# A gated linear-attention and MLP kernel on one core: the scores move onto two 64-row tiles of TensorE, the state update alternates column halves, and k is loaded without its zeroed half

## The reference

```
m_new = max(f + m, i);  f_stab = exp(f + m - m_new);  i_stab = exp(i - m_new)
C = f_stab * C + i_stab * outer(v, k)      # 40 x 40 state per head
n = f_stab * n + i_stab * k
y = sigmoid(o) * (C q) / max(|n . q|, 1)
```

```
h  = relu(x^T @ w_tok1) @ w_tok2;  u = x + h^T
x2 = u + relu(u @ w_ch1) @ w_ch2                 # 320 -> 1536 -> 320
out = (sigmoid(conv5(x2)) * (x2 @ w_val)) @ w_out
```

## Time and profile before

| | us |
|---|---|
| median of three runs | 288.86 |
| profiled execution, whole | 291.4 |
| its span, first to last instruction | 289.3 |
| TensorE busy | 264.7 (91%) |
| VectorE busy | 180.0 (62%) |
| ScalarE busy | 115.4 (40%) |
| GpSimd busy | 85.7 (30%) |

### The profile page before, as it was taken

How to read it: one execution, slowest core, us unless ns; L and a number is a source line. 1 busy time by engine, 2 the same in 40 slices (tenths; PEclk the granted TensorE clock), 3 DMA queues, 4 the chain that set the end, 5 groups by cost and what they waited for, 6 DMA issues and landing times.

```text
span 289.3 us, 5204 instructions
## 1 busy us (share of the span) xinstructions
PE 264.7 (91%) x1964; PEld 247.3 (85%) x1964; DVE 180.0 (62%) x401; ACT 115.4 (40%) x212; POOL 85.7 (30%) x102
## 2 busy tenths in 40 slices
PE   0598788999999999999999999999999999999675
PEld 0587677679799999999999997899999999999564
DVE  7988877486878568535866303537653168742991
ACT  2664545488444432443432223322232332232731
POOL 4415578903654553155004000000040000130710
PEclk9999999999999999999999999999999999999988
DMA  7699987664765143220000010000000100000101
GB/s 219 155 274 321 302 265 219 212 198 124 208 189 132 57 142 91 84 68 3 0 0 2 3 66 2 0 0 2 0 2 23 45 1 2 0 2 0 56 13 68
DMA packets 26289, 25.68 MB, mean 89 GB/s; under 512 B 13977, under 2 KB 22009, under 8 KB 26265
## 3 DMA queue, kind: packets, MB, share of 16 engines
q1 hardware_dynamic: 21976, 18.72, 22.2%
q10 hardware_dynamic: 4288, 6.64, 7.1%
HBM read 23.34 MB, written 2.02 MB: 88 GB/s over the span
## 4 chain that ended last, share of the span: by engine, by line
PE 74%; DVE 7%; issue 7%; POOL 5%; ACT 4%; DMA 1%; SPq 0%; ACTq 0%; POOLq 0%; DVEq 0%
PE shared L1172 30%; PE h_ps L1306 22%; PE s_ps L1210 4%; PE hv_ps L1191 2%; PE s_ps L1244 2%; PE hv_ps L1195 2%; DVE gate L1039 2%; PE shared L1271 2%; PE h_ps L1244 2%; POOL qs L597 2%; PE shared L1221 1%; DMA mask_sb<-mask 1%; PE shared L1318 1%; DVE prob L930 1%; PE shared L1256 1%
## 5 line engine op out<-in xcount | busy, mean ns | idle before, releaser
L1104 DVE SCALAR_TENSOR_TENSOR h_lo<-shared,h_hi 128x384 fp32r<-128x384 f32 x48 | 26.5, 557 | 40.2 <-ACT h_hi L824 40.1
L1306 PE MATMUL h_ps<-ch_hi,h_hi 128*128 128x320 f32 x144 | 45.4, 315 | 0.0
L1306 PE MATMUL h_ps<-ch_hi,h_lo 128*128 128x320 f32 x144 | 44.5, 309 | 0.0
L824 ACT ACTIVATE h_hi<-shared 128x384 fp32r<-128x384 f32 x48 | 23.1, 488 | 53.2 <-PE shared L1172 50.1
L1306 PE MATMUL h_ps<-ch_lo,h_hi 128*128 128x320 f32 x144 | 44.3, 308 | 0.0
L1172 PE MATMUL shared<-u_hi,ch_hi 128*128 128x384 f32 x96 | 33.1, 344 | 0.1
L1172 PE MATMUL shared<-u_lo,ch_hi 128*128 128x384 f32 x96 | 32.6, 339 | 0.0
L1172 PE MATMUL shared<-u_hi,ch_lo 128*128 128x384 f32 x96 | 32.5, 339 | 0.0
L1210 PE MATMUL s_ps<-q_in,k_in 128*128 128x128 f32 x192 | 27.1, 300 | 3.9 <-DMA q_in<-qT 3.9
L1210 PEld LDWEIGHTS s_ps<-q_in,k_in 128*128 128x128 f32 x192 | 25.2, 211 | 6.1 <-DMA q_in<-qT 4.5
L1039 DVE SCALAR_TENSOR_TENSOR gate<-x,conv_sb,gate 128x384 f32<-128x384 f32 x44 | 29.0, 668 | 1.0
(11 more groups left out here) (181 smaller groups left out, 550.3 us busy)
## 6 DMA issues: line engine op xcount, KB each, us to landing
G_all<-G_scratch SPq DMA_DIRECT2D x11, 512.0 KB, 5.8
o_sig<-on ACTq DMA_DIRECT2D x2, 960.0 KB, 6.7
k_in<-kT SPq DMA_DIRECT2D x24, 80.0 KB
q_in<-qT SPq DMA_DIRECT2D x24, 80.0 KB
kn_in<-kn SPq DMA_DIRECT2D x12, 160.0 KB, 4.3
v_in<-vn SPq DMA_DIRECT2D x12, 160.0 KB, 4.8
stage<-ch ACTq DMA_DIRECT2D x3, 640.0 KB, 4.3
out<-o_sb SPq DMA_DIRECT2D x12, 160.0 KB, 1.8
```

The source lines that it names most:

```text
L824: act.activation(h_hi[i % 3][:], ps_of(key)[:, 0:T], ACT.Relu).then_inc(hi_ready, 1)
L1104: took(dve.scalar_tensor_tensor(out=h_lo[i % 3][:], in0=ps_of(key)[:, 0:T], scalar=0.0, in1=h_hi[i % 3][:].bitcast(F32), op0=ALU.max, op1= ...
L1306: last = pe.matmul(h2_ps[t][:, 0:DM], a[:, tile_cols(t)], w[:, f, :], start=(f == 0 and n == 0), stop=(f == FT - 1 and n == 2))
```

## The change

The scores lose the zeroed half: k_in becomes 128 x 512 like q_in, and a score matmul reads only its group's 40 rows (partitions 0 to 39 or 64 to 103) of k and q. The groups alternate, j outer and g inner, and each group still has its own bank. Both banks are now waited for at once, on TensorE before the first score matmul and on VectorE before the first product. The delta matmuls alternate between the output halves 0 to 63 and 64 to 103 in the same way. kn of the last chunk of a batch (u = 5 and 11), which nothing reads, is not loaded. The two memsets of k_in go, and the first k is issued before the wait for `zeroed`. Both k_in buffers now have room of their own, so k uses them in turn for all chunks.

```diff
-        k_in = [sb("k_in0", [P, 2, HG * L]), sb("k_in1", [P, 2, HG * L], at=a_at + 4 * S)]
+        k_in = [sb(f"k_in{k}", [P, HG * L]) for k in range(2)]
...
-        def k_buffer(u):
-
-            return 1 if u < NC and u % 2 else 0
-
-        def k_users(u):
-
-            return [x for x in range(u + 1) if k_buffer(x) == k_buffer(u)]
+        def kn_users(u):
+
+            return [x for x in range(u % 2, u + 1, 2) if x % NC < NC - 1]
...
             def k_chunk(u):
-                users = k_users(u)
-                if len(users) > 1:
-
-                    sp.wait_ge(s_ready, 2 * (users[-2] + 1))
+                if u >= 2:
+
+                    sp.wait_ge(s_ready, 2 * (u - 1))
                 for g in range(2):
-                    sp.dma_start(k_in[k_buffer(u)][64 * g:64 * g + D, g, :],
-                                 kT[u, g]).then_inc(k_loaded[k_buffer(u)], 16)
+                    sp.dma_start(k_in[u % 2][64 * g:64 * g + D, :], kT[u, g]).then_inc(k_loaded[u % 2], 16)
...
-                kn_chunk(u)
+                if u % NC < NC - 1:
+                    kn_chunk(u)
                 v_chunk(u)
...
-            sp.wait_ge(zeroed, 4)
             k_chunk(0)
+            sp.wait_ge(zeroed, 2)
             q_chunk(0)
...
-            pool.memset(k_in[1][:], 0.0).then_inc(zeroed, 1)
...
-            dve.memset(k_in[0][:], 0.0).then_inc(zeroed, 1)
...
                 if n < NC:
+                    dve.wait_ge(s_ready, 2 * u + 2)
                     for g in range(2):
                         w = 2 * u + g
                         dve.wait_ge(exp_ready, w + 1)
-                        dve.wait_ge(s_ready, w + 1)
                         dve.tensor_tensor(prob[w % 4][:], s_ps[g][:], prob[w % 4][:], ALU.mult).then_inc(prob_ready, 1)
...
-                    for g in range(2):
-                        w = 2 * u + g
-                        if w >= 2:
-                            pe.wait_ge(prob_ready, w - 1)
-                        for j in range(HG):
-                            last = pe.matmul(s_ps[g][:, tile_cols(j)], k_in[k_buffer(u)][:, g, tile_cols(j)],
-                                             q_in[k][:, tile_cols(j)], start=True, stop=True)
-                        last.then_inc(s_ready, 1)
+                    if u >= 1:
+                        pe.wait_ge(prob_ready, 2 * u)
+                    for j in range(HG):
+                        for g in range(2):
+                            r = slice(64 * g, 64 * g + D)
+                            last = pe.matmul(s_ps[g][:, tile_cols(j)], k_in[k][r, tile_cols(j)],
+                                             q_in[k][r, tile_cols(j)], start=True, stop=True)
+                            if j == HG - 1:
+                                last.then_inc(s_ready, 1)
...
-                    for h in range(H):
-                        g, j = divmod(h, HG)
-                        m = 64 if g == 0 else D
-                        last = pe.matmul(ps[64 * g:64 * g + m, j * D1:(j + 1) * D1],
-                                         kn_in[k][:, h * D:h * D + m], wv[:, h, :], start=True, stop=True)
+                    for j in range(HG):
+                        for g in range(2):
+                            h = g * HG + j
+                            m = 64 if g == 0 else D
+                            last = pe.matmul(ps[64 * g:64 * g + m, j * D1:(j + 1) * D1],
+                                             kn_in[k][:, h * D:h * D + m], wv[:, h, :], start=True, stop=True)
```

More of the change, by code:

```diff
@@ L449, in kn_chunk @@
                 t0 = (u % NC) * L
-                if u >= 2:
-                    full(sp, ("delta", u - 2 if (u - 2) % NC < NC - 1 else u - 3))
+                users = kn_users(u)
+                if len(users) > 1:
+                    full(sp, ("delta", users[-2]))
                 sp.dma_start(kn_in[u % 2][:], kn[u // NC, t0:t0 + L, :]).then_inc(kn_loaded[u % 2], 16)
@@ L1203, in attention @@
                     pe.wait_ge(q_loaded[k], 32 * (u // 2 + 1))
-                    pe.wait_ge(k_loaded[k_buffer(u)], 32 * len(k_users(u)))
-                    for g in range(2):
-                        w = 2 * u + g
-                        if w >= 2:
-                            pe.wait_ge(prob_ready, w - 1)
-                        for j in range(HG):
-                            last = pe.matmul(s_ps[g][:, tile_cols(j)], k_in[k_buffer(u)][:, g, tile_cols(j)],
-                                             q_in[k][:, tile_cols(j)], start=True, stop=True)
-                        last.then_inc(s_ready, 1)
+                    pe.wait_ge(k_loaded[k], 32 * (u // 2 + 1))
+                    if u >= 1:
[7 more added lines that the diff above has]
+                                last.then_inc(s_ready, 1)
                 if n < NC - 1:
@@ L1216, in attention @@
                     pe.wait_ge(wv_ready, with_next(u))
-                    pe.wait_ge(kn_loaded[k], 16 * (u // 2 + 1))
-                    for h in range(H):
-                        g, j = divmod(h, HG)
-                        m = 64 if g == 0 else D
-                        last = pe.matmul(ps[64 * g:64 * g + m, j * D1:(j + 1) * D1],
-                                         kn_in[k][:, h * D:h * D + m], wv[:, h, :], start=True, stop=True)
+                    pe.wait_ge(kn_loaded[k], 16 * len(kn_users(u)))
+                    for j in range(HG):
[4 more added lines that the diff above has]
+                                             kn_in[k][:, h * D:h * D + m], wv[:, h, :], start=True, stop=True)
                     last.then_inc(shared_full, 1)
```

## The result

The changed kernel is slower: 294.45 us median (293.94 to 296.52, 4 runs) against 288.62 us (288.04 to 289.34, 4 runs) of the kernel before on the same chip. The ratio is 1.0214 with a 95% interval of 1.0159 to 1.0269. The profiled execution has a span of 292.1 us and took 293.94. Some executions of a kernel are slower than its others at a lower clock, and the ratios leave out those over 1.5% above its fastest.

A forecast was written before the change was run, and what follows sets the result against it. TensorE, 91% busy, was taken as the bound, except around chunk 7's exponents on VectorE. Batch 1's shift, batch 0 and the clock gave 2.6 - 0.2 + 0.6 = +3.0 on 288.86: 291.9 us, range 286.3 to 295.2.

The forecast's parts named there:

- batch 0, up to chunk 6: Batch 0: hv(5) waits less because VectorE's second product comes 0.2 us earlier; -0.2, with ends -1.0 and +0.8.
- chunk 7's collision: Chunk 7: GpSimd's early wv, kept, qs and L543 hold VectorE's exponents, moving delta(7) from 77.80 to 81.0; +3.2 us.
- chunk 8 (collision, then clock): Chunk 8: GpSimd beside the exponents makes VectorE's path 9.9 us against 9.75 before; shift reaches +3.4.
- chunk 9: Chunk 9: later L543 work delays and holds exponents, path 12.0 us against 10.5 before; shift reaches +4.9.
- chunk 10: Chunk 10: no L543 here, so 10.0 us against 10.5 before; shift falls to +4.4.
- chunk 11: Chunk 11: state(10) comes 0.76 us sooner after the product and scores save 1.0; shift falls to +2.6, staying to the end.
- The clock: Behind the hole before delta(7), 4.5 us long: a clock fall may lose up to 1.7 us; half of 1.2 taken, +0.6.
- The faster rival: Batch 1: early GpSimd work harms nothing and the shorter scores pay; -3.6, 285.3 us; chance 0.19.
- GpSimd against VectorE: Batch 1's exponents: each GpSimd instruction holds one exponent for its length, and one gets through between two of them.
- Row tiles don't pair: Scores keep 1.78 us and VectorE's first product starts 0.9 late, beside the collisions; near +5.5, 294.9 us; chance 0.09.
- Cancel: Batch 1: half the collision in chunk 7, those in 8 to 10 within VectorE's idle time; 288.5 us; chance 0.12.

The follow-up runs named there:

- early v with the wait: Kernel before with v of chunks 7 to 10 issued right behind G, and GpSimd's wv waiting for its chunk's exponents: 288.74 us, ratio 0.9978.
- early v alone: Kernel before with one edit, v of chunks 7 to 10 issued directly behind G, ahead of k: 295.20 us, ratio 1.0194.
- k one back: Changed kernel with k from chunk 7 on again waiting for the scores of the chunk before: 289.61 us median of four, too wide for a ratio.
- the filler: Changed kernel with 40 junk matmuls between scores(7) and delta(7): 293.41 us, ratio 1.0136.
- the version without collision: Changed kernel with GpSimd's wv waiting for its chunk's exponents in batch 1, and batch 0's scores one group after the other: 287.26 us, ratio 0.9923.
- the changed kernel with the wait: Changed kernel with GpSimd's wv in batch 1 waiting for VectorE's eight exponents of that chunk: 287.51 us, ratio 0.9924.

## Why the prediction was right, and what it mis-sized

Forecast 291.9 us, range 286.3 to 295.2; measured 294.45. The mechanism was the predicted one, and the size was too small by 2.5 us. Most signs below "what would show it" came: wv without a wait for v_in; exponents of chunk 7 at 6.9 us (6.7 predicted), chunk 8 at 4.8 (4.6), chunk 9 at 6.6 (6.6); delta(7) waiting 4.66 us (4.5). Two signs didn't come, and both go against the prediction's own sums. The sixteen scores take 1.16 us and not 0.9 to 1.0, though their saving from start to delta is 0.89 (1.98 to 1.09), as forecast (0.90): the sign left out the 0.2 of tail and change of shape. And chunk 9's exponents are not the longest.

The shift of the first product, step by step. It is the row of after minus the row of before, at chunks 6 to 11: -0.8, +2.6, +4.8, +6.0, +5.4, +4.3.

| step | predicted | measured |
|---|---|---|
| batch 0, up to chunk 6 | -0.2 | -0.8 against the profiled before, +0.2 against early v with the wait |
| chunk 7's collision | +3.2 | +3.4 |
| chunk 8 (collision, then clock) | +0.2, clock +0.6 | +2.2, of which the clock 1.8 |
| chunk 9 | +1.5 | +1.2 |
| chunk 10 | -0.5 | -0.6 |
| chunk 11 | -1.8 | -1.1 |

The total needs a better row to compare with. The profiled execution of the kernel before was late for reasons of its own; early v with the wait runs the same TensorE instructions, and its profiled execution (288.69) lies at its median. Against that one the profiled kernel before comes 1.0 us later from 49 to 274 us and 2.4 later at its end, and the changed kernel 5.3 later at chunk 11 and 5.2 later at the end, close to the 5.8 of the medians; from chunk 7 on the steps are those of the table. So it is luck that the forecast of the span, 292.3, meets the measured 292.1: it stood on a late execution, and the shift was 3.0 where over 5 came. Of what was missing, chunk 8 has 1.4, chunk 11 0.7 and batch 0 0.4.

*The clock* is the step that was mis-sized most. The prediction took half of a 1.2 us loss; the fall came and cost 1.84 us at chunk 8's product, which waited 1.85 for scores, where VectorE had been reckoned to be the late one. The reckoning of 1.7 at most, "of which 0.5 is hidden by state(7)", assumed 3.4 us at 0.50; the rows show 4.0 us at 0.50 and 4.0 at 0.73, 3.1 us of full speed. The fall came in all three profiled kernels with an unfilled hole of 3.8 to 4.7 us before delta(7): 0.50, 0.50 and 0.65 in 80 to 84 us (the change, early v alone, k one back), so half was too low a chance. How much of it reaches the end is less sure: 0.4 us by chunk 11 in the traces, where the filler let a second fall in, 1.0 by the medians, 0.8% by the ratios.

*Chunk 11* regained 1.1 and not 1.8. The step took 0.8 for state coming sooner and 1.0 for shorter scores in one interval; the version without collision shows that interval at 9.53 us where the kernel before had 10.53, which is 1.0 in all. The prediction had said itself that a first product doesn't gain by the scores right before it. The faster rival's -3.6 is too large as well: freed of the collision the change is worth 2.9 us by the spans (284.0 against the 286.9 of early v with the wait) and 1.5 by the medians (287.26 against 288.74). Chunk 8's first product doesn't gain (86.92 against 86.89), those of 9 to 11 gain 0.8, 0.8 and 1.0 more each.

*Batch 0* gave -0.8 in the traces, but the profiled execution of before was itself late there: the two kernels with early v, whose batch 0 runs the same instructions, have this product at 69.51 and 69.74 and the changed one at 69.72. The gain of 0.2 that was forecast is not to be seen. The clock was lower at 36 to 40 us (0.71 in the changed kernel, 1.00 before), but that alone doesn't explain it: at 1.00 there, two versions with batch 0's scores by groups have the product at 69.50 and 69.58.

*From chunk 11 to the end* the profiled execution of before took another 1.5 us more than the changed one. The fall of the clock of the earlier trace rows lies there (so the 0.994 given ahead of the prediction is the mean granted clock; it was full but for these 3.4 us), and the changed one stayed at 1.00 in those stretches; that the fall is all of the 1.5 isn't shown, since early v with the wait had 0.70 in 275 to 280 us and was not late. So the spans differ by 2.8 where the medians differ by 5.8. The prediction had noted that the profiled execution stood above the median but laid the difference on both kernels alike.

*GpSimd against VectorE.* Sum right, picture too even. The prediction let one exponent through between any two GpSimd instructions. In the raw records one exponent, started at 74.69, was held for 3.26 us by kept, qs and the low part together, and none got through between them. In the end three exponents were left, as reckoned. The Trainium skill's page "SBUF — State Buffer" ("SBUF: two separate sides") calls the shared port pair an exclusive lock held per instruction, which the experiment with one added wait agrees with: 6.90 us with, 3.50 without GpSimd beside them.

*Rivals.* "Row tiles don't pair" is refuted by 1.16 against 2.05 us, and by the pairs of starts, which are the row that the prediction lacked; its own terms add to 5.7, not 5.5. "The early work harms nothing" needed wv to start after the exponents; where a wait forces that, the kernel is faster than before, by 0.8%, less than the 285.3 us that the rival named. "Cancel" needed half a collision, and chunk 7's was full.

## What to carry to other kernels

A wait that looks like waste may be what keeps two engines apart. Before freeing a queue, ask which instructions will start earlier, on which engine, and what runs beside them; here GpSimd's wait on data was worth 1.9% of the kernel before (early v alone), and once the change had removed it, an explicit wait on the other engine's work (one line) brought 2.9%, more than was lost (287.5 and 287.3 us in its two versions, the best medians of this study, against some 289 before). Read a hole in TensorE's work by what it does to the clock behind it too: the unfilled ones of 3.8 to 4.7 us here were each followed by 0.50 to 0.65. Junk matmuls can only help if they can run inside the hole (those that stood behind it added 3.95 us), and here filling one hole was followed by a fall behind the next.

## What the runs showed of the hardware beside this

Matmuls on two row tiles of 40 rows run side by side when they alternate: sixteen in 1.16 us. In the order of the groups they take 1.71, still less than the full array's 2.05. The raw starts show why: around the change of group three instructions start 4 to 7 ns from a neighbour, and all others stand alone, 0.11 us apart, so some pairing happens there by itself. In column halves the same holds in small: delta 0.66 alternating, 0.76 by halves.

In batch 0 the clock fell in some profiled executions and not in others of nearly the same program: 0.50 in 36 to 40 us in the changed kernel with the wait, 1.00 in the version with batch 0's scores one group after the other, 0.67 when ten matmuls were added in chunk 7 (in this order; columns as in the earlier trace rows):

```profile
36.00:40.00 4.00, 4.00 (x36) 3.51 (x36) 3.50 (x14) 1.78 (x3) 3.67 (x4) 0.50 0.89 244
```

```profile
36.00:40.00 4.00, 3.98 (x45) 3.02 (x44) 3.67 (x15) 2.04 (x4) 3.17 (x5) 1.00 0.90 261
```

```profile
36.00:40.00 4.00, 3.37 (x44) 3.11 (x41) 3.85 (x14) 1.60 (x3) 4.00 (x5) 0.67 0.89 248
```

Scores of 1.71 us in batch 0 don't prevent it: of the five profiled kernels that have them with the wait, two show it. What decides it stays open.
